# An own order of TensorE's work for the last three tiles ahead of the experts

## The reference

```
# attention: pooled by 4, plus local (|i - j| < 4)
out_d = softmax(scale * q_d @ k_d.T) @ v_d            # q_d, k_d, v_d: means of 4 rows
out_local = softmax(where(|i-j| < 4, scale * q @ k.T, -1e9)) @ v
x = repeat(out_d, 4) + out_local                      # (1152, 512)
# mixture of 8 experts, each with capacity 288
logits = x @ w_gate; e = argmax(logits); gate = softmax(logits)[e]
slot of token i = number of earlier tokens with the same expert; kept if < 288
y = gate * relu(x @ w1[e]) @ w2[e]                    # w1: 512x1024, w2: 1024x512
# feed-forward with mish
h = y @ w_in; out = (h * tanh(softplus(h))) @ w_out   # 512x2048, 2048x512
```

## Time and profile before

| | us |
|---|---|
| median of 3 runs | 470.04 |
| lowest and highest run | 466.25, 472.26 |
| the profiled execution's own time | 470.12 |
| its span, first to last instruction | 468.0 |
| TensorE busy | 444.5 (95% of the span) |
| vector engine busy | 279.8 (60%) |
| ScalarE busy | 229.7 (49%) |
| GpSimd busy | 137.7 (29%) |
| TensorE's share of the chain that ended last | 81% |

### The profile page before, as it was taken

The page is one execution under the profiler, slowest core; times in us unless marked ns, Lnnn a source line. Parts: engine busy times, 40 slices in busy tenths (PEclk is TensorE's granted clock), DMA queues, the critical chain, the costliest instruction groups (busy, mean ns, idle before and its releaser), DMA issues.

```text
span 468.0 us, 10181 instructions
## 1 busy us (share of the span) xinstructions
PE 444.5 (95%) x3428; PEld 409.4 (87%) x3429; DVE 279.8 (60%) x665; ACT 229.7 (49%) x631; POOL 137.7 (29%) x136
## 2 busy tenths in 40 slices
PE   8899898898799999999999999999999999999994
PEld 8678787788799999999999889998899889998972
DVE  7888587857110110111111799888888888888873
ACT  2767666713223333323324666555755556655541
POOL 9685634101000000000004566322453233532202
PEclk9999999979999999999999999999999999999999
DMA  9999999231898998986765224121141211321001
GB/s 185 199 197 158 190 364 388 91 112 59 319 323 273 344 334 264 336 298 219 248 220 163 62 45 90 45 90 47 49 154 45 88 46 46 125 78 45 1 0 67
DMA packets 72144, 74.97 MB, mean 160 GB/s; under 512 B 32817, under 2 KB 47921, under 8 KB 72113
## 3 DMA queue, kind: packets, MB, share of 16 engines
q1 hardware_dynamic: 70384, 69.84, 51.3%
q0 software_dynamic: 1728, 4.72, 2.6%
HBM read 65.11 MB, written 9.44 MB: 159 GB/s over the span
## 4 chain that ended last, share of the span: by engine, by line
PE 81%; DVE 7%; ACT 5%; issue 3%; DMA 3%; POOL 0%; POOLq 0%; SPq 0%; ACTq 0%; DVEq 0%
PE ps L1178 76%; ACT pr L707 3%; DMA xg<-x_by_expert 2%; PE ps L1432 1%; DMA x_by_expert<-x_sb,xslot 1%; PE ps L1308 1%; PE ps L1262 1%; DVE sme L939 1%; DVE mx L932 1%; PE ps L1257 0%; DVE sme L928 0%; PE ps L1203 0%; DVE qdT L891 0%; DVE kdT L891 0%; ACT xT L690 0%
## 5 line engine op out<-in xcount | busy, mean ns | idle before, releaser
L641 POOL TENSOR_TENSOR wiL<-raw,wiH 128x512 fp32r<-128x512 f32 x48 | 62.5, 1304 | 249.5 <-ACT wiH L690 146.3
L1178 PE MATMUL ps<-xe,raw 128*128 128x128 f32 (+2 forms) x512 | 70.3, 298 | 3.9 <-issue 2.5
L1178 PEld LDWEIGHTS ps<-xe,raw 128*128 128x128 f32 x512 | 68.9, 191 | 5.0 <-issue 2.9
L1178 PE MATMUL ps<-hid,raw 128*128 128x128 f32 (+2 forms) x512 | 70.8, 297 | 0.0
L1178 PEld LDWEIGHTS ps<-hid,raw 128*128 128x128 f32 x512 | 69.0, 191 | 0.0
L1178 PE MATMUL ps<-x2H,wiH 128*128 128x384 f32 x192 | 65.1, 339 | 0.3 <-DVE x2L L1084 0.3
L1178 PE MATMUL ps<-x2L,wiH 128*128 128x384 f32 x192 | 65.3, 340 | 0.0
L1178 PE MATMUL ps<-x2H,wiL 128*128 128x384 f32 x192 | 64.6, 337 | 0.0
L1178 PE MATMUL ps<-woH,gH 128*128 (+1 forms) x144 | 56.9, 395 | 2.5 <-DVE gL L1084 2.5
L1178 PE MATMUL ps<-woH,gL 128*128 (+1 forms) x144 | 57.2, 397 | 0.0
L1178 PE MATMUL ps<-woL,gH 128*128 (+1 forms) x144 | 56.7, 394 | 0.0
(11 more groups left out here) (140 smaller groups left out, 765.0 us busy)
## 6 DMA issues: line engine op xcount, KB each, us to landing
raw<-in_moe_w SPq DMA_DIRECT2D x32, 1024.0 KB, 7.6
raw<-in_moe_w_in SPq DMA_DIRECT2D x24, 512.0 KB, 3.6
x_by_expert<-x_sb SPq DMA_DIRECT2D x1, 4608.0 KB, 16.4
xg<-x_by_expert SPq DMA_DIRECT2D x8, 512.0 KB, 3.7
wo_in<-in_moe_w_out SPq DMA_DIRECT2D x8, 512.0 KB
v<-in_v SPq DMA_DIRECT2D x4, 576.0 KB
qk_tok<-in_k SPq DMA_DIRECT2D x8, 256.0 KB, 4.8
qk_tok<-in_q SPq DMA_DIRECT2D x8, 256.0 KB, 5.2
```

Of the source, the lines that this page charges most:

```text
L641: nc.gpsimd.tensor_tensor(wiL[:, r, :, :], raw_wi_tile(r), wiH[:, r, :, :].bitcast(F32), ALU.subtract).then_inc(s_wil, 1)
L1178: return T.matmul(out_, a, b, start=start, stop=stop, skip_group_check=True)
```

## The change

TensorE's loop now ends with round 14, and a function `last_tiles` gives the rest in an order of its own: the attend of the last step comes ahead of the turn of tile 7, the turned probabilities of the last tile ahead of tile 6's logits, the turn of tile 8 ahead of tile 7's logits, and the counts of tile 7 between the two halves of `early_rows`. The turned x of tile 7 goes to bank 3 and that of tile 8 to bank 1 (`x_bank`), tile 8's copy in SBUF to the half of `pr` that is free (`x_turned`), and tile 8's logits to bank `XB` (`lg_bank`). The waits follow: the turns of tiles 7 and 8 wait for all exponentials (`s_exp`) in place of the logits copy before them, and the logits of tile 7 wait for the logits copy of tile 6. ScalarE copies the turned x of tile 7 at the end of round 16, behind the copy of tile 8's x, in place of at its beginning. The vector engine's order stays as it is.

```
--- before.py
+++ after.py
@@ -329,6 +329,20 @@
 
             return n - LAG_X - 1 if 0 <= n - LAG_X - 1 < NT else None
 
+        def x_bank(t):
+
+            return {NT - 2: 3, NT - 1: 1}.get(t, TB)
+
+        def x_turned(t):
+
+            if t == NT - 1:
+                return pr[:, 1, :, :].rearrange("p a w -> p (a w)")[:, 0:K1 * P]
+            return xT[:, :]
+
+        def lg_bank(t):
+
+            return XB if t == NT - 1 else TB
+
         def count_turn(n):
 
             return n - LAG_X - 2 if 0 <= n - LAG_X - 2 < NT else None
@@ -732,9 +746,11 @@
 
             def xt_copy(t):
                 act.wait_ge(s_xt, t + 1)
-                if t >= 1:
+                if t == NT - 1:
+                    act.wait_ge(s_pt, NS - 1)
+                elif t >= 1:
                     act.wait_ge(s_lg, t)
-                copy(xT[:, :], ps[:, TB, :]).then_inc(s_xtc, 1)
+                copy(x_turned(t), ps[:, x_bank(t), :]).then_inc(s_xtc, 1)
 
             def gate_exp(t):
 
@@ -745,7 +761,7 @@
                 k_copy(t)
             act.wait_ge(s_cb, 5)
             for n in range(ROUNDS):
-                if x_turn(n) is not None:
+                if x_turn(n) is not None and x_turn(n) != NT - 2:
                     xt_copy(x_turn(n))
                 if count_turn(n) is not None and n < ROUNDS - 1:
                     gate_exp(count_turn(n))
@@ -760,6 +776,8 @@
                 for m in attended(n):
                     if is_local(m) and m != n - 2:
                         x_copy(m)
+                if x_turn(n) == NT - 2:
+                    xt_copy(NT - 2)
 
             def xe_copy(e, c):
 
@@ -977,7 +995,7 @@
 
                 c = slice(t, t + 1)
                 dve.wait_ge(s_lg, t + 1)
-                V.tensor_copy(lg[:, t, :], ps[:, TB, 0:E]).then_inc(s_lgc, 1)
+                V.tensor_copy(lg[:, t, :], ps[:, lg_bank(t), 0:E]).then_inc(s_lgc, 1)
                 dve.wait_ge(s_lgc, t + 1)
                 link(V.tensor_reduce(r_mx[:, c], lg[:, t, :], X, ALU.max))
                 V.tensor_scalar(lgd[:, t, :], lg[:, t, :], r_mx[:, c], None, ALU.subtract).then_inc(s_lgd, 1)
@@ -1302,18 +1320,22 @@
 
             def x_transpose(t):
                 pe.wait_ge(s_avc, RANK[local_step(t)] + 1)
-                if t >= 1:
+                if t >= NT - 2:
+                    pe.wait_ge(s_exp, NS)
+                elif t >= 1:
                     pe.wait_ge(s_lgc, t)
                 for c in range(K1):
-                    last = T.transpose(ps[:, TB, c * P:(c + 1) * P], x_sb[:, t, c * P:(c + 1) * P], ident)
+                    last = T.transpose(ps[:, x_bank(t), c * P:(c + 1) * P], x_sb[:, t, c * P:(c + 1) * P], ident)
                 last.then_inc(s_xt, 1)
 
             def logits(t):
                 pe.wait_ge(s_xtc, t + 1)
                 if t == 0:
                     pe.wait_ge(s_wg, 16)
+                if t == NT - 2:
+                    pe.wait_ge(s_lgc, t)
                 for c in range(K1):
-                    last = mm(ps[:, TB, 0:E], xT[:, c * P:(c + 1) * P], wg[:, c, :], c == 0, c == K1 - 1)
+                    last = mm(ps[:, lg_bank(t), 0:E], x_turned(t)[:, c * P:(c + 1) * P], wg[:, c, :], c == 0, c == K1 - 1)
                 last.then_inc(s_lg, 1)
 
             pe.wait_ge(s_warm, 1)
@@ -1351,6 +1373,8 @@
                 pe.wait_ge(s_xg0, 16)
                 pe.wait_ge(s_rc, 2 * NT - 4)
                 for c in range(K1):
+                    if c == K1 // 2:
+                        counts(ROUNDS - 2)
                     for r0 in range(0, FULL, P):
                         mm(ps[:, c, r0:r0 + P], xg[:, r0 // P, c * P:(c + 1) * P], ident, r0 == 0, False)
 
@@ -1363,27 +1387,26 @@
                     if t == NT - 1:
                         last.then_inc(s_xet, 1)
 
-            for n in range(ROUNDS):
-                if n < NS:
-                    if count_turn(n - 2) is not None:
-                        pe.wait_ge(s_rc, 2 * count_turn(n - 2) + 2)
-                    if n >= 2:
-                        pe.wait_ge(s_exp, n - 1)
-                    if n == FIRST_DOWN[0]:
-                        keep_warm_in_turns(2 * (n % 2), WARM_SUMS, TURN_WAIT)
-                    if n in FIRST_DOWN:
-                        pe.wait_ge(s_qd, HELD + 1 if n == FIRST_DOWN[0] else NT)
-                    if turned(n - 1) == NT - 1:
-                        pe.wait_ge(s_qTc, NT)
-                    if is_local(n):
-                        pe.wait_ge(s_qTc, STEPS[n][1] + 1)
-                        pe.wait_ge(s_kTc, min(STEPS[n][1] + 2, NT))
-                    if 0 < n < FIRST_DOWN[1] and not (is_local(n) and STEPS[n][1] >= HELD):
-                        if is_down(n):
-                            keep_warm_in_turns(2 * (n % 2), WARM_DOWN, TURN_DOWN)
-                        else:
-                            keep_warm_in_turns(2 * (n % 2), WARM_LOCAL, TURN_LOCAL)
-                    scores(n)
+            for n in range(NS):
+                if count_turn(n - 2) is not None:
+                    pe.wait_ge(s_rc, 2 * count_turn(n - 2) + 2)
+                if n >= 2:
+                    pe.wait_ge(s_exp, n - 1)
+                if n == FIRST_DOWN[0]:
+                    keep_warm_in_turns(2 * (n % 2), WARM_SUMS, TURN_WAIT)
+                if n in FIRST_DOWN:
+                    pe.wait_ge(s_qd, HELD + 1 if n == FIRST_DOWN[0] else NT)
+                if turned(n - 1) == NT - 1:
+                    pe.wait_ge(s_qTc, NT)
+                if is_local(n):
+                    pe.wait_ge(s_qTc, STEPS[n][1] + 1)
+                    pe.wait_ge(s_kTc, min(STEPS[n][1] + 2, NT))
+                if 0 < n < FIRST_DOWN[1] and not (is_local(n) and STEPS[n][1] >= HELD):
+                    if is_down(n):
+                        keep_warm_in_turns(2 * (n % 2), WARM_DOWN, TURN_DOWN)
+                    else:
+                        keep_warm_in_turns(2 * (n % 2), WARM_LOCAL, TURN_LOCAL)
+                scores(n)
                 if turned(n) is not None:
                     t = turned(n)
                     if n:
@@ -1396,8 +1419,6 @@
                     transpose_q(t)
                 if x_turn(n) is not None:
                     x_transpose(x_turn(n))
-                if NS <= n < ROUNDS - 2 and count_turn(n) is not None:
-                    counts(n)
                 if n == local_step(HELD) + 1:
                     pe.wait_ge(s_kTc, NT)
                     keep_warm_in_turns(TB, WARM_PROBS, TURN_WAIT)
@@ -1406,17 +1427,31 @@
                         attend(m)
                 if x_turn(n) is not None:
                     logits(x_turn(n))
-                if n == ROUNDS - 2:
-                    early_rows()
-                if n >= ROUNDS - 2:
-                    counts(n)
                 if n == 1:
                     pe.wait_ge(s_qTc, 2)
-                if 0 <= n - 1 < NS:
+                if n >= 1:
                     probs_t(n - 1)
                 for m in attended(n):
                     if m != n - 2:
                         attend(m)
+
+            def last_tiles():
+
+                x_transpose(NT - 3)
+                counts(NS)
+                attend(NS - 2)
+                probs_t(NS - 1)
+                logits(NT - 3)
+                attend(NS - 1)
+                x_transpose(NT - 2)
+                counts(NS + 1)
+                x_transpose(NT - 1)
+                logits(NT - 2)
+                logits(NT - 1)
+                early_rows()
+                counts(ROUNDS - 1)
+
+            last_tiles()
 
             def three(out_, aH, aL, bH, bL, first, last_):
```

## The result

Over 20 runs each, before takes 470.55 us (466.25 to 475.16) and the changed kernel 467.76 us (463.95 to 475.80) in the median; the ratio is 0.9933, with a 95% interval of 0.9906 to 0.9960. That is 3.2 us (1.9 to 4.4) less, where 3.5 us less was forecast. Every ratio here is one of the runs within 1.5% of their kernel's fastest, the medians are of all runs.

A forecast was written before the change was run, and what follows sets the result against it. The prediction took the vector engine's order-caused waits, passed on through scatters and expert loads to TensorE, to bound the kernel. Slots, tables and loads 3.5 us earlier gave 470.1 - 3.5 = 466.6 us, range 464.2 to 470.6.

The forecast's parts named there:

- the vector engine's two waits: Before the change, 2.25 us for tile 8's logits and 2.15 us for tile 7's counts; both forecast to go.
- The way there: Chain from late tiles' slots through GpSimd's last scatter and expert 0's and 1's loads to TensorE at 120.41 us.
- The step-by-step schedule: Forecast start times from the last attend at 91.51 us to the first hidden matmul at 104.8 us.
- the tables: Expert tables, ready 1.60 us before the first hidden matmul and taken to help start it; forecast 3.5 us earlier.
- The slot named in the chain: Vector engine's slots of the late tiles, ending at 105.51 us before; forecast at 101.9 to 102.0.
- the sum's base: The forecast sum, 470.1 - 3.5 = 466.6 us, started from a trace with low clock from 95.2 to 102.0 us.
- I take the full clock: Assumed full clock over the new stretch: 3.5 us gained, 466.6 us, chance 0.45.
- tighter packing: Work ahead of 95.2 us loses idle times of 0.2, 0.35 and 0.69 us, so the clock should stay full.
- The first rival: Clock falls as before at the same place, over the early rows: gain 1.75 us, 468.4 us, chance 0.30.
- The second: Low clock comes later, over the late rows and expert 0: 470 to 471.7 us, chance 0.13.
- the point of decision: Length of the later low stretch, 7.0 us, from which that rival decides the outcome.
- The cold branch: TensorE's 2.31 us wait at 125.08 us may be hidden or recur: 464.3 or 469.1 us, chance 0.12.

The follow-up runs named there:

- before_again: The kernel before, unchanged, run for a second trace; the clock was again low over the early rows.
- before_third: The kernel before, unchanged, run for a third trace; the clock was again low over the early rows.
- counts_ahead_only: The kernel before with only tile 7's counts moved ahead of the early rows; ratio 1.0051 (1.0006 to 1.0096).
- before_warm: The kernel before, same order, with 5 unused small matmuls ahead of tile 8's turn and 9 behind it; median 468.25 us, ratio 0.9992.

## Why the prediction was right, and where it was not

**The time** was forecast as 466.6 us, and 467.76 us was measured, inside the range of 464.2 to 470.6 and on the forecast side. That the first measurement's 3.2 us lie so near the forecast 3.5 us is in part luck: the later ones gave ratios of 0.9999 and 1.0018, and at the same low time the change is worth 1.0 us.

**What bounds the kernel** was right: the vector engine's two waits are in part an effect of order (1.24 and 0.43 us are left of them at full clock in the old order, none in the new), and what is won up to the turn of expert 1's rows goes to the end: from that turn to the end of the span are 347.6, 347.2 and 347.7 us in the three traces of before, 347.7, 346.8 and 347.5 in those of the changed kernel. The way there is only in part the one of the earlier trace rows: in before_again and before_third TensorE did not wait for the load of expert 1's rows, and the turn followed the first hidden matmul by 10.8 and 11.4 us.

**The step-by-step schedule** was right to 0.1 us up to the early rows, and nearly so behind them. Counts of tile 7 were forecast at 11.0 (98.4) and read at 10.67; the first hidden matmul, forecast at 17.4 (104.8), came at 16.94 in the trace at full clock, 3.94 us earlier than in the first trace of before where 3.5 were forecast. In before the first hidden matmul came 0.84 us behind the end of the late rows; in all five traces of the changed kernel, with and without warm-up matmuls, it follows them with no idle time, so there TensorE's late rows, and no longer the tables, set its start. The slot named in the chain is tile 7's; the last one, tile 8's, ends 0.38 us behind it, in both kernels.

**The mis-sized term is the sum's base.** The prediction took a trace of before with a low clock over the early rows and, for the new order, "I take the full clock", and booked the whole 3.5 us on the change. By the experiments it is two terms: the order at equal clock is worth 1.19 us in the traces (1.0 us in the runs), and the step from low to full clock is worth 2.74 us at the slots, which the old order shows too once its clock is full; together 3.93. That the order brings that step is not shown. For it: in this stretch the low time was 6.8 us in each trace of before, 3.4, 3.4 and 0 in those of the changed kernel. Against it: the mean low time of whole runs is the same, and counts_ahead_only and before_warm reached full clock in the old order of the tiles. The prediction's argument that tighter packing keeps the clock did not hold as a rule; in two of three traces the clock fell all the same, later.

**The first rival**, low as before at the same place, was seen in no trace of the changed kernel as it was forecast. **The second**, a later low stretch, was seen in two of three, over part of the early and of the late rows, 3.4 us long and not 7.0: hidden matmul at 18.41 for 16.94, 1.47 us lost. It cost 0.43 of its length where one half was forecast, and did not reach the point of decision. **The cold branch** stayed on the path in every trace; the wait ahead of expert 1's first hidden matmul was 1.6 to 3.5 us, so it scatters by more than the order is worth. It is a branch: in each of the 13 traces the longest one on TensorE's queue in this stretch (1.83 to 3.66 us) is 0.1 to 0.2 us longer than the wait. The reading that it is a load of code rests on the Trainium skill ("Runtime: NRT & Kernel Launch", "Instruction fetch mechanics"), which gives no duration for it; no run here tested it.

**Open**: why the first 20 runs showed 3.2 us, when the later ratios mean 0.0 us less and 0.8 us more, and the means of all runs, with no run left out, 1.1 and 0.8 us less (2.0 us in the first 20). The changed kernel's low time in that first batch was 12.4 us in the mean, as later; that of before is not known, so a difference in clock cannot be shown there.

## What to carry to other kernels

Before pricing a change from one trace, ask which clock the stretch had and price both kernels at the same one; here a low stretch of 6.8 us was worth 2.7 us at the slots, the reordering 1.2. A cheap way to see the order alone is to fill TensorE's idle times with small matmuls in both kernels, and to fit the run times against the time at low clock. Where one engine waits on another's order, the bank that two steps share is the first thing to free: here no other part was worth as much (1.32 us of 0.50 to 1.32).

## What the runs showed of the hardware

The clock fell over the same piece of work, tile 8's logits and the early rows, in three of three traces of before, although TensorE's longest idle time just ahead of the fall was 0.35 us. A low stretch was 3.4, 6.8 or 13.7 us long (apart from one that was still open at the end of each trace), and a run had 1 to 28 us of them in all; each low microsecond cost 0.42 us of time. The same scatter of x rows took from 2.7 to 4.8 us from its start to the issue of the load that waits for it.
